# Regrouping six PSUM banks in a fused attention and expert kernel: three for transposed scores, three for raw scores

## What is computed

```python
# attention: 4 x 8 heads, 576 positions, 64 wide
scores = scale * (q @ k.T) + cum[:, None] - cum[None, :]     # cum = cumsum(log(clip(f, 1e-4, 1)))
scores = where(causal, -1e9, scores)
attn = softmax(scores); x = (attn @ v), heads side by side   # (2304, 512)
# dense layer
h = x @ w_in; g = where(h >= 1, h, where(h <= -1, 0, (h + 1)**2 / 4)); x = g @ w_out
# one expert of 8 for each row, by cosine similarity
out[row] = gate[row] * (relu(x[row] @ w1[e]) @ w2[e])
```

## Time and profile before

| what | us |
|---|---|
| median of 3 runs (lowest, highest) | 856.62 (856.4, 856.82) |
| the profiled execution | 856.74 |
| its span, first to last instruction | 854.5 |
| PE busy | 835.6 (98% of the span) |
| PE weight loads busy | 781.9 (91%) |
| DVE busy | 411.4 (48%) |
| ACT busy | 395.5 (46%) |
| POOL busy | 351.1 (41%) |

### The profile page before, as it was taken

How to read it: one execution, slowest core, us unless ns; L and a number is a source line. 1 busy time by engine, 2 the same in 40 slices (tenths; PEclk the granted TensorE clock), 3 DMA queues, 4 the chain that set the end, 5 groups by cost and what they waited for, 6 DMA issues and landing times.

```text
span 854.5 us, 13804 instructions
## 1 busy us (share of the span) xinstructions
PE 835.6 (98%) x5018; PEld 781.9 (91%) x5019; DVE 411.4 (48%) x1002; ACT 395.5 (46%) x916; POOL 351.1 (41%) x366
## 2 busy tenths in 40 slices
PE   8999999999999999999999999999999999999996
PEld 5888888889999999999999999999998998998985
DVE  6877888787554454444444445455525210210201
ACT  6777777777665534534534544443332121211221
POOL 5665678773766211111102201084311592010285
PEclk9999999999999999999999999999999999999999
DMA  6676888872100201211031023242323354213041
GB/s 223 192 222 221 261 276 264 277 218 75 56 1 1 102 30 55 84 47 56 17 101 41 29 102 105 74 149 62 85 76 111 110 161 135 82 42 124 26 138 40
DMA packets 70941, 95.62 MB, mean 112 GB/s; under 512 B 7174, under 2 KB 47110, under 8 KB 70864
## 3 DMA queue, kind: packets, MB, share of 16 engines
q1 hardware_dynamic: 62688, 80.33, 30.6%
q10 hardware_dynamic: 6416, 9.59, 3.2%
q0 software_dynamic: 1760, 4.72, 1.5%
HBM read 70.87 MB, written 24.27 MB: 111 GB/s over the span
## 4 chain that ended last, share of the span: by engine, by line
PE 91%; ACT 4%; DVE 1%; issue 1%; DMA 1%; SPq 0%; POOL 0%; POOLq 0%; ACTq 0%
PE psum L1508 24%; PE psum L1510 24%; PE psum L1509 24%; PE psum L1479 5%; PE psum L1462 5%; PE psum L1435 4%; ACT pr L848 2%; ACT pth L858 2%; PE psum L1440 1%; DVE ptl L1118 1%; DMA qraw<-q 1%; PE psum L1591 1%; PE psum L1575 0%; PE psum L1576 0%; PE psum L1415 0%
## 5 line engine op out<-in xcount | busy, mean ns | idle before, releaser
L1508 PE MATMUL psum<-xh,winh 128*128 128x384 f32 x384 | 129.1, 336 | 0.0
L1508 PE MATMUL psum<-gh,wouth 128*128 128x384 f32 x384 | 128.3, 334 | 0.2 <-issue 0.2
L1509 PE MATMUL psum<-xl,winh 128*128 128x384 f32 x384 | 128.4, 334 | 0.0
L1510 PE MATMUL psum<-xh,winl 128*128 128x384 f32 x384 | 128.4, 334 | 0.0
L1510 PE MATMUL psum<-gh,woutl 128*128 128x384 f32 x384 | 128.3, 334 | 0.0
L1509 PE MATMUL psum<-gl,wouth 128*128 128x384 f32 x384 | 128.3, 334 | 0.0
L882 ACT ACTIVATE hpos<-psum,minus 128x384 f32<-128x384 f32 x96 | 55.9, 582 | 142.3 <-DVE hclip L1144 142.1
L1149 DVE TENSOR_TENSOR g<-hpos,hsq 128x384 f32<-128x384 f32 x96 | 64.7, 674 | 109.0 <-ACT hsq L884 109.0
L675 POOL TENSOR_TENSOR xst<-xst 128x384 f32<-128x384 f32 x24 | 24.6, 1025 | 175.6 <-DMA xst<-rinv_d 175.6
L1254 DVE SCALAR_TENSOR_TENSOR hl<-psum,hh 128x384 fp32r<-128x384 f32 x48 | 26.8, 557 | 139.5 <-ACT hh L938 139.5
L1153 DVE TENSOR_TENSOR gl<-g,gh 128x384 fp32r<-128x384 f32 x96 | 64.1, 668 | 61.0 <-ACT gh L915 61.0
(11 more groups left out here) (233 smaller groups left out, 1863.5 us busy)
## 6 DMA issues: line engine op xcount, KB each, us to landing
praw<-moe_w SPq DMA_DIRECT2D x48, 256.0 KB, 2.7
qraw<-q SPq DMA_DIRECT2D x15, 448.0 KB, 4.6
vraw<-vk SPq DMA_DIRECT2D x16, 320.0 KB, 3.4
xh<-yh_d SPq DMA_DIRECT2D x20, 256.0 KB, 4.2
xl<-yl_d SPq DMA_DIRECT2D x20, 256.0 KB, 4.5
kraw<-k SPq DMA_DIRECT2D x16, 288.0 KB, 3.7
xa_d<-xo SPq DMA_DIRECT2D x16, 288.0 KB, 3.9
xb_d<-xo SPq DMA_DIRECT2D x16, 288.0 KB, 4.2
```

The source lines that it names most:

```text
L1508: nc.tensor.matmul(psum_at, ah, bh, start=start, stop=False)
L1509: nc.tensor.matmul(psum_at, ah, bl, start=False, stop=False)
L1510: return nc.tensor.matmul(psum_at, al, bh, start=False, stop=stop)
```

## The change

Of the six banks, three go to fills and three to scores.

- `PT = (3, 4, 5)`: fill k of pair p takes bank `PT[(8 * p + k) % 3]`, so it waits for the low part of the fill three back, not two. `of_bank`, `turn_inverse` and `copy_turned` follow.
- `score_banks` deals banks 0 to 2 to the blocks, block 8 getting two neighbouring ones. `minimum_ahead` gives the wait: a block now waits for the minimum three slots back, not four. For block 8 that is block 6 (before: block 5), for block 1 it is block 8 of the pair before (before: block 7), for block 3 it is block 0.
- `MASK_LATER = (1, 4)`: block 1's mask is issued behind block 2's products.
- DVE's loop loses its exception: the minimum of block 1 is taken in its own step, which puts it behind the low parts of fills 2 and 3.
- The dense layer's first two units wait for one more minimum each (`STEPS - 1 + u`).

```diff
-        PT, PX, PY = (4, 5), 6, 7
+        SCORES, PT, PX, PY = 3, (3, 4, 5), 6, 7
...
+        def score_banks(p, i):
+            if i == NB - 1:
+                return (p % 2, p % 2 + 1)
+            return (((0, 2, 1), (2, 0, 1))[p % 2][i % SCORES],)
+        def minimum_ahead(p, i):
+            last = (NB + 1) * p + i + (i == NB - 1) - SCORES
+            return NB * (last // (NB + 1)) + min(last % (NB + 1), NB - 1) + 1 if last >= 0 else 0
...
+        def fill_bank(p, k):
+            return PT[(FILLS * p + k) % len(PT)]
...
             for n in range(-AHEAD, STEPS + TAIL):
-                m = tile_of(n + 3)[1]
-                if m != 1 and 0 <= n + 3 < STEPS:
+                if 0 <= n + 3 < STEPS:
                     masked(n + 3)
-                if m == 0 and 0 <= n + 4 < STEPS:
-                    masked(n + 4)
...
-            MASK_LATER = (4,)
+            MASK_LATER = (1, 4)
...
-                last = 10 * p + i + (i == NB - 1) - 4
-                if last >= 0:
-                    pe.wait_ge(lowest, NB * (last // 10) + min(last % 10, NB - 1) + 1)
+                if minimum_ahead(p, i):
+                    pe.wait_ge(lowest, minimum_ahead(p, i))
...
-                if FILLS * p + k >= 2:
-                    pe.wait_ge(pt_l, FILLS * p + k - 1)
-                if k == 1 and p >= 2:
+                if FILLS * p + k >= len(PT):
+                    pe.wait_ge(pt_l, FILLS * p + k - len(PT) + 1)
+                if k == len(PT) - 1 and p >= 2:
                     pe.wait_ge(r_copied, p - 1)
...
-                        pe.wait_ge(lowest, STEPS - 2 + u)
+                        pe.wait_ge(lowest, STEPS - 1 + u)
```

More of the change, by code:

```diff
@@ L375, in stacked, with of_bank @@
             return bass.AP(full.tensor, full.offset, [[full.ap[0][0], P], [ROW, nb], [1, ni * P]])
-        def of_bank(k):
+        def fill_bank(p, k):
+            return PT[(FILLS * p + k) % len(PT)]
+        def of_bank(p, k):
             _, b, nb, i, ni = FILL[k]
-            full = psum[:, PT[k % 2], 0:nb * ni * P]
+            full = psum[:, fill_bank(p, k), 0:nb * ni * P]
             return full if nb == 1 or i < 4 else full.rearrange("p (b c) -> p b c", b=nb)
@@ L857, in high @@
                 rows = D if k == FILLS - 1 else P
-                nc.scalar.copy(stacked(pth, k)[0:rows], of_bank(k)[0:rows]).then_inc(pt_h, 1)
+                nc.scalar.copy(stacked(pth, k)[0:rows], of_bank(p, k)[0:rows]).then_inc(pt_h, 1)
             def copy_early(p):
@@ L1087, in masked @@
                     dve.wait_ge(exped, NB * (p - 1))
-                bank = (10 * p + i) % 4
+                banks = score_banks(p, i)
                 out_at, c_at = pr[:, at_tile(i):at_tile(i) + w], c8[:, p % 2, 0:w]
                 if i < NB - 1:
-                    src = psum[:, bank, 0:w]
+                    src = psum[:, banks[0], 0:w]
                 else:
-                    src = psum[:, bank:bank + 2, 0:w // 2]
+                    src = psum[:, banks[0]:banks[1] + 1, 0:w // 2]
                     out_at = out_at.rearrange("p (a c) -> p a c", a=2)
@@ L1114, in low @@
                     last = stacked(pth, k)
-                    nc.vector.tensor_tensor(last[D:P], of_bank(k)[0:D], last[0:D].bitcast(F32),
+                    nc.vector.tensor_tensor(last[D:P], of_bank(p, k)[0:D], last[0:D].bitcast(F32),
                                             ALU.subtract).then_inc(pt_l, 1)
                 else:
-                    nc.vector.tensor_tensor(stacked(ptl, k), of_bank(k), stacked(pth, k).bitcast(F32),
+                    nc.vector.tensor_tensor(stacked(ptl, k), of_bank(p, k), stacked(pth, k).bitcast(F32),
                                             ALU.subtract).then_inc(pt_l, 1)
@@ L1123, in copy_turned @@
                     dve.wait_ge(r_out[p % 2], 16 * (p // 2))
-                nc.vector.tensor_copy(rturn[:, p % 2, :], psum[0:NB, PT[1], P:2 * P]).then_inc(r_copied, 1)
+                nc.vector.tensor_copy(rturn[:, p % 2, :], psum[0:NB, fill_bank(p + 1, FILLS - 1), P:2 * P]).then_inc(r_copied, 1)
             def copy_late_a(p):
@@ L1405, in _ @@
                                  ident_b[:].unsqueeze(1).to_broadcast([P, 4, P]), start=True, stop=True)
-            MASK_LATER = (4,)
+            MASK_LATER = (1, 4)
             def mask(n):
                 p, i = tile_of(n)
-                bank, w = (10 * p + i) % 4, keys(i)
+                bank, w = score_banks(p, i)[-1], keys(i)
                 if i == NB - 1:
-                    bank, w = bank + 1, w // 2
+                    w = w // 2
                 nc.tensor.matmul(psum[:, bank, w - D:w], ident_b[:], mask_b[:], start=False,
@@ L1425, in score @@
                     pe.wait_ge(q_l, p + 1)
-                last = 10 * p + i + (i == NB - 1) - 4
-                if last >= 0:
-                    pe.wait_ge(lowest, NB * (last // 10) + min(last % 10, NB - 1) + 1)
-                bank = (10 * p + i) % 4
+                if minimum_ahead(p, i):
+                    pe.wait_ge(lowest, minimum_ahead(p, i))
+                banks = score_banks(p, i)
                 passes = ((qh, kh), (qh, kl), (ql, kh))
                 if i < RAW:
-                    nc.tensor.matmul(psum[:, bank, 0:w], qf[:, p % 2, i, :], kf[:, p % 2, 0:w], start=True, stop=False)
+                    nc.tensor.matmul(psum[:, banks[0], 0:w], qf[:, p % 2, i, :], kf[:, p % 2, 0:w], start=True, stop=False)
                 elif i < NB - 1:
                     for a, (q_, k_) in enumerate(passes):
-                        nc.tensor.matmul(psum[:, bank, 0:w], q_[:, p % 2, i - RAW, :], k_[:, p % 2, 0:w],
+                        nc.tensor.matmul(psum[:, banks[0], 0:w], q_[:, p % 2, i - RAW, :], k_[:, p % 2, 0:w],
                                          start=a == 0, stop=False)
@@ L1439, in score @@
                         for a, (q_, k_) in enumerate(passes):
-                            nc.tensor.matmul(psum[:, bank + j, 0:w // 2], q_[:, p % 2, i - RAW, :],
+                            nc.tensor.matmul(psum[:, banks[j], 0:w // 2], q_[:, p % 2, i - RAW, :],
                                              k_[:, p % 2, j * (w // 2):(j + 1) * (w // 2)],
@@ L1461, in turn @@
                         at = (b - b0) * ni + i - i0
-                        x = nc.tensor.transpose(psum[:, PT[k % 2], at * P:(at + 1) * P],
+                        x = nc.tensor.transpose(psum[:, fill_bank(p, k), at * P:(at + 1) * P],
                                                 pr[:, at_tile(i) + b * P:at_tile(i) + (b + 1) * P], ident[:])
@@ L1469, in turn_inverse @@
                 pe.wait_ge(inv_ok, p + 1)
-                return nc.tensor.transpose(psum[:, PT[1], P:2 * P], rinv[:, p % 2, :], ident[:])
+                return nc.tensor.transpose(psum[:, fill_bank(p + 1, FILLS - 1), P:2 * P], rinv[:, p % 2, :], ident[:])
             def head(p, h, i0, ni, dst, signal):
```

## The result

| | before | after |
|---|---|---|
| median, us | 856.72 | 849.82 |
| lowest to highest | 856.4 to 857.6 (4 runs) | 849.31 to 850.06 (4 runs) |
| profiled execution | 856.74 | 849.58 |
| its span | 854.5 | 847.4 |

A forecast was written before the change was run, and what follows sets the result against it. Fill stalls cost PE 1.15 us a pair; a loop of waits through block 8 would then bound pairs at 11.65. Saving 13 x 0.56 + 0 + 0.5 = 7.8 us gave 848.8 on the median's footing, range 845.0 to 852.8.

The forecast's parts named there:

- the loop: Waits from block 8 over PE, ACT and DVE back to it: no pair shorter than 11.65 us, against 12.21 before.
- PE's own 11.06: PE's time for a middle pair without its fill stalls: 12.21 - 1.15 = 11.06 us.
- the x split: Part of DVE's 3.72 us from low part 6 to minimum 6, without idle; pairs without it at most 0.05 shorter.

## What to carry over

A stall that ends at a buffer is priced by what closes next: write down the loop from a wait over all engines and back to it, and sum its rows; that length is the floor until the loop itself is shortened or opened, and behind it stands the next loop (here 11.59, then 11.43, then PE's own 11.06). A buffer taken from another use closes loops that were open. When the loop decides, order inside it is worth as much as a buffer: here putting four casts ahead of two exponentials gave 6.5 us, the banks 6.9. And take each term of such a loop from all repeats of its instruction: in the kernel before, seven of the eight pairs show 0.70 to 0.73 for the x split and would have misled as one did, while the same line in the dense layer took 0.55 (291.43), with nothing on POOL. For an instruction with two SBUF inputs look at what POOL runs beside it.

## What the hardware showed

- A DVE subtraction of two SBUF tiles (128x384) takes 0.54 us alone. When POOL is on one of its splits, it ends 0.40 to 0.42 behind the end of POOL's instruction, in the four pairs shown and in all 80 of the 104 x splits of these 13 traces that took 0.63 or more; it was up to 2.28. The profile shows no idle time for it: the row itself is long.
- It goes the other way too: POOL's qh, 0.94 otherwise, took 1.50 when DVE's split ran at the same time (119.04 and 119.19), and ended 0.81 behind DVE's end.
- A small one is caught as well. In the kernel after, the denominators' 128x9 operation, 0.17 in ten of the thirteen middle pairs, took 1.05 when it began together with POOL's step on the x tile (and 1.04 in the next pair, in the same way):

```profile
102.67 1.05 DVE L1118 TENSOR_SCALAR rden<-rsum 128x9 f32<-128x9 f32 x1
```
```profile
102.67 1.02 POOL L691 TENSOR_TENSOR xst<-xst 128x384 f32<-128x384 f32 x1
```

It ends 0.03 behind POOL. It makes low part 4 late, and fill 7 lost 0.1 more in these two pairs; neither is longer than its like. In the first middle pair the operation took 1.16, beside POOL's split of v, and fill 7 lost 0.2 more.
